# A linear-attention kernel fused with two feed-forward layers: the normed unit is transposed at the end of TensorE's step, the state's sum and decay move in halves

## What is computed

```
scale = min(|a|, 0.999) / (|a| + 1e-6),  a_n = a * scale      (a complex)
S = a_n[t] * S + k[t] v[t]^T ;   y[t] = q[t] . Re S
x  = y, heads side by side: 3072 rows of 384
xn = x / sqrt(mean(x*x) + 1e-6) * g
x2 = (silu(xn @ w_gate) * (xn @ w_val)) @ w_out               (384 -> 1536 -> 384)
out = softplus(x2 @ w_in) @ w_out2                            (384 -> 2048 -> 384)
```

## Time and profile before

| | |
|---|---|
| median of 3 runs | 1287.45 us (1284.30 to 1287.48) |
| profiled execution, its own time | 1289.8 us |
| its span, first to last instruction | 1288.1 us |
| TensorE matmul busy | 1117.6 us (87%), 5495 instructions |
| TensorE weight load busy | 940.5 us (73%) |
| VectorE busy | 751.8 us (58%), 2204 instructions |
| ScalarE busy | 617.9 us (48%) |
| GpSimd busy | 307.4 us (24%) |
| granted TensorE clock, mean | 0.965 of full speed |
| DMA queues, share of 16 engines | 24.2% |

### The profile page before, as it was taken

How to read it: one execution, slowest core, us unless ns; L and a number is a source line. 1 busy time by engine, 2 the same in 40 slices (tenths; PEclk the granted TensorE clock), 3 DMA queues, 4 the chain that set the end, 5 groups by cost and what they waited for, 6 DMA issues and landing times.

```text
span 1288.1 us, 18819 instructions
## 1 busy us (share of the span) xinstructions
PE 1117.6 (87%) x5495; PEld 940.5 (73%) x5495; DVE 751.8 (58%) x2204; ACT 617.9 (48%) x1136; POOL 307.4 (24%) x260
## 2 busy tenths in 40 slices
PE   0444469999999899989898999998999999999996
PEld 0444457777777777777777788887888888888885
DVE  7788878798888798889889841121222222222211
ACT  2233334444444444444444433345666666666664
POOL 0023331111111111111111111464333333333332
PEclk9999998898999899999899899999999999999999
DMA  2444442242333323333332230232010101010000
GB/s 70 118 134 129 130 117 55 75 122 79 88 104 93 91 70 113 91 85 96 95 99 83 68 93 1 77 119 87 1 50 1 50 1 50 0 49 0 24 1 25
DMA packets 63850, 91.22 MB, mean 71 GB/s; under 512 B 4624, under 2 KB 53648, under 8 KB 63760
## 3 DMA queue, kind: packets, MB, share of 16 engines
q1 hardware_dynamic: 63760, 90.15, 24.2%
HBM read 60.89 MB, written 29.24 MB: 70 GB/s over the span
## 4 chain that ended last, share of the span: by engine, by line
issue 30%; PE 26%; DVE 19%; DMA 11%; POOL 9%; SPq 2%; ACT 1%; DVEq 1%; POOLq 0%; ACTq 0%
PE gbank L1303 13%; POOL pl L539 9%; DVE prep L819 8%; DMA rows_scratch<-pk 6%; DMA mm<-rows_scratch 5%; DVE pk L819 4%; PE xbank L1332 3%; PE xbank L1331 3%; PE ybank L1303 3%; PE xbank L1335 2%; SPq L336 1%; DVE xn L1039 1%; PE sbank L1343 1%; DVE state L1002 1%; DVE at L1009 1%
## 5 line engine op out<-in xcount | busy, mean ns | idle before, releaser
L1303 PE MATMUL gbank<-xh,slab 128*128 128x512 f32 x1296 | 426.0, 411 | 1.9 <-issue 1.9
L1303 PE MATMUL ybank<-ph,slab 128*128 128x512 f32 x1020 | 319.2, 394 | 4.9 <-ACT ytile L645 4.0
L1303 PEld LDWEIGHTS gbank<-xh,slab 128*128 128x128 f32 x1296 | 255.4, 200 | 55.1 <-issue 2.1
L1303 PE MATMUL gbank<-xl,slab 128*128 128x512 f32 x648 | 262.2, 405 | 0.0
L514 POOL TENSOR_TENSOR pl<-hid,ph 128x512 fp32r<-128x512 f32 x72 | 107.3, 1490 | 535.9 <-ACT ph L638 535.9
L1303 PEld LDWEIGHTS ybank<-ph,slab 128*128 128x128 f32 x1020 | 189.3, 189 | 43.0 <-issue 5.6
L1303 PE MATMUL ybank<-pl,slab 128*128 128x512 f32 x510 | 199.3, 391 | 0.0
L539 POOL TENSOR_TENSOR pl<-hid,ph 128x512 fp32r<-128x512 f32 x96 | 125.7, 1309 | 267.0 <-ACT ph L756 267.0
L1187 DVE SCALAR_TENSOR_TENSOR hid<-gbank,hid 128x512 f32<-128x512 f32 x72 | 49.8, 691 | 214.4 <-ACT hid L747 214.4
L1303 PEld LDWEIGHTS gbank<-xl,slab 128*128 128x128 f32 x648 | 128.6, 198 | 29.1
L1050 DVE TENSOR_TENSOR hid<-gbank,hid 128x512 f32<-128x512 f32 x72 | 49.7, 691 | 115.7 <-PE gbank L1303 112.8
(11 more groups left out here) (124 smaller groups left out, 1561.9 us busy)
## 6 DMA issues: line engine op xcount, KB each, us to landing
rows_scratch<-pk SPq DMA_DIRECT2D x24, 771.0 KB, 5.0
mm<-rows_scratch SPq DMA_DIRECT2D x96, 192.8 KB, 4.0
a_in<-in_a SPq DMA_DIRECT2D x24, 384.0 KB, 5.3
kq_in<-in_kq SPq DMA_DIRECT2D x24, 384.0 KB, 4.9
ytile<-in_w SPq DMA_DIRECT2D x36, 192.0 KB, 4.3
prep<-in_w SPq DMA_DIRECT2D x32, 192.0 KB, 2.6
y_scratch<-ytile SPq DMA_DIRECT2D x7, 768.0 KB, 5.8
v_in<-in_v SPq DMA_DIRECT2D x24, 192.0 KB, 4.6
```

The source lines that it names most:

```text
L1303: last = pe.matmul(out, slab[:, slot + part, cols], x, start=f, stop=l)
```

## The change

Six edits, on four engines:

1. **TensorE:** `xt_of(x)` moves from before `outputs(m, 0)` to before `outputs(m, 1)`. It now waits for `mask(m, 1)`, and `scores(m, 0)` instead of `scores(m, 1)` waits for `x_low` (of the step before).
2. **ScalarE:** `xh_of` moves to match, from before `y_copy(m, 0)` to before `y_copy(m, 1)`, behind `hi(3i + 2)`. **VectorE:** `x_low` moves from before `p_of(3i + 2)` to just before `keys`.
3. **VectorE:** `decay` is split in halves of four heads. `decay(m, 0)` stands before `total`, `decay(m, 1)` before `scaled_frame`; each waits for its own half of `mm`, and `outputs(m, hf)` for its own half.
4. **VectorE:** `state_add(m, 1)` moves from the end of a step into the next one, behind `limits(n)`.
5. **VectorE:** `p_of(3i + 1)` moves ahead of `mask(m, 0)`, `sum_of(n + 1)` some ten operations forward, `query` ahead of `p_of(3i + 2)`, `mask(m, 1)` ahead of `odd`, and the small operations of the norm one place back each.
6. **SyncE:** `load_a(n + 1)` moves from behind `load_kq(n)` to between the two halves of `load_mm`.

What is stored in `pk`, `mm` and the scratch is the same as before. The core of the diff:

```diff
@@ SyncE, step
                     load_mm(m, 0, 1 - par)
+                if n is not None and not (isinstance(n, int) and n + 1 >= NU):
+                    load_a(n + 1)
+                if m is not None:
                     load_mm(m, 1, 1 - par)
...
                 if w1 is not None:
-                    load_a(n + 1)
                     load_w1(w1 + 1)
@@ ScalarE, step
-                if x is not None:
-                    xh_of(x, par, col, T)
                 if m is not None:
                     y_copy(m, 0)
...
+                if x is not None:
+                    xh_of(x, par, col, T)
                 if m is not None:
                     y_copy(m, 1)
@@ VectorE
-            def decay(m):
-                dve.wait_ge(mm_loaded[0], 32 * (m + 1))
-                dve.wait_ge(mm_loaded[1], 32 * (m + 1))
-                need(dve, s_added, 2 * m)
-                dve.tensor_tensor(state[:, :, :], state[:, :, :],
-                                  mm[:, :, 2 * CH:2 * CH + 1].broadcast_to([2 * D, H, D]), ALU.mult).then_inc(decayed, 1)
+            def decay(m, hf):
+                dve.wait_ge(mm_loaded[hf], 32 * (m + 1))
+                need(dve, s_added, 2 * m + hf - 1)
+                heads = slice(hf * HH, (hf + 1) * HH)
+                dve.tensor_tensor(state[:, heads, :], state[:, heads, :],
+                                  mm[:, heads, 2 * CH:2 * CH + 1].broadcast_to([2 * D, HH, D]), ALU.mult).then_inc(decayed, 1)
@@ TensorE
             def scores(m, hf):
                 need(pe, masked, 2 * m + hf)
-                if hf:
-                    pe.wait_ge(xl_done, m + 1)
+                if not hf:
+                    need(pe, xl_done, m)
...
-                pe.wait_ge(decayed, m + 1)
+                pe.wait_ge(decayed, 2 * m + hf + 1)
...
-                pe.wait_ge(masked, 2 * m + 1 if m is not None else 2 * NU)
+                pe.wait_ge(masked, 2 * (m + 1) if m is not None else 2 * NU)
@@ TensorE, step
-                if x is not None:
-                    xt_of(x, m)
                 if m is not None:
                     outputs(m, 0)
...
                     out_block(T, 3 * i + 2)
+                if x is not None:
+                    xt_of(x, m)
                 if m is not None:
                     outputs(m, 1)
```

More of the change, by code:

```diff
@@ L369, in step @@
                 if w1 is not None:
-                    load_a(n + 1)
                     load_w1(w1 + 1)
                     load_w1(w1 + 2)
-                elif n is not None and not (isinstance(n, int) and n + 1 >= NU):
-                    load_a(n + 1)
                 if n is not None:
@@ L1063, in step @@
                     limits(n)
+                if m is not None and not (isinstance(m, int) and m == 0):
+                    state_add(m - 1, 1)
+                if n is not None:
                     scale(n)
@@ L1078, in step @@
                     total_products(n)
+                if m is not None:
+                    decay(m, 0)
+                if n is not None:
                     total(n)
+                if T is not None:
+                    p_of(T, 3 * i + 1)
+                if n is not None:
                     after_products(n, 1)
@@ L1082, in step @@
                     mask(m, 0)
-                    decay(m)
                 if n is not None:
@@ L1087, in step @@
                     x_mean(x)
-                    x_first(x)
                 if n is not None:
                     after_products(n, 2)
+                if n is not None and not (isinstance(n, int) and n + 1 >= NU):
+                    sum_of(n + 1)
                 if x is not None:
-                    x_second(x)
+                    x_first(x)
                 if n is not None:
@@ L1096, in step @@
                 if x is not None:
-                    x_root(x)
+                    x_second(x)
                 if n is not None:
@@ L1101, in step @@
                 if x is not None:
-                    x_norm(x)
+                    x_root(x)
                 if n is not None:
@@ L1106, in step @@
                     end_root(n)
[L1107 to L1110, removed]
+                if x is not None:
+                    x_norm(x)
                 if n is not None:
@@ L1113, in step @@
                     after_sums(n, 8)
+                if T is not None and i == 0:
+                    y_out(T)
+                if n is not None:
                     turn_of(n)
@@ L1116, in step @@
                     frame_sums(n)
-                if T is not None and i == 0:
-                    y_out(T)
+                if m is not None:
+                    decay(m, 1)
                 if n is not None:
@@ L1123, in step @@
                     carry_of(n)
+                    last(n)
                 if m is not None:
@@ L1126, in step @@
                 if n is not None:
-                    last(n)
                     middle_products(n)
+                    query(n)
                     middle(n)
-                if x is not None:
-                    x_low(x, par, col)
                 if T is not None:
@@ L1135, in step @@
                     odd_products(n)
-                    query(n)
-                    odd(n)
                 if m is not None:
@@ L1140, in step @@
                 if n is not None:
+                    odd(n)
                     even_products(n)
                     even(n)
+                if x is not None:
+                    x_low(x, par, col)
+                if n is not None:
                     keys(n, 0)
@@ L1146, in step @@
                     queries(n, 1)
-                if m is not None:
-                    state_add(m, 1)
             def x2_low(T, par):
```

## The result

| | before | after |
|---|---|---|
| median | 1287.17 us (4 runs, 1284.30 to 1287.48) | 1211.08 us (4 runs, 1208.93 to 1212.67) |
| ratio | | 0.9412, 95% interval 0.9392 to 0.9433 |
| profiled execution, span | 1288.1 us | 1209.8 us |
| granted clock, mean | 0.965 | 0.994 |
| TensorE matmul busy | 1117.6 us | 1080.2 us |

The account below looks back on a forecast made before the run. TensorE was held by waits and a lowered clock, with VectorE the next bound at 28.0 us a lap. Terms summed to -79.6 us from 1289.8, giving 1210.2; less 2.35 for the median, 1208 us, range 1190 to 1240.

Parts of the forecast that it names:

- The wait for `xn` goes, and the clock comes back: TensorE, second stage: wait before the transposes goes, 1.7 us per lap on average; clock gives back up to 41.7 us.
- The first rival: Part is given back: clock still falls once per lap or the square lands no earlier; laps 29.5, 1235 us; chance 0.25.
- VectorE becomes the bound at 28.0 us a lap: Second stage: VectorE's own work 27.6 us, plus 0.06 for split decay and 0.3 of wait, sets the lap.
- the 0.3 us for `sum_of`: VectorE: the earlier sum_of(n + 1) waits 0.3 us per lap for ScalarE's square of a; bounds 0 and 1.8 us.
- TensorE waits 1.3 us for `mm` in each lap: TensorE at kt_of(m, 0): its 26.7 us lap against VectorE's 28.0 leaves a wait of 1.3 us.
- The last unit costs 2 us: Last unit, no attention to follow: transposes come at the step's end and tile 5 waits for copy and remainder, +2 us.
- The first stage: Four laps fall from 32.82 to 28.9 us: both state_add waits go, a wait of 0.8 for mask(m, 0) comes; -15.7 us.
- moves cost nothing by themselves: VectorE: reordering its operations adds no time of its own to the lap; only the second decay instruction adds 0.06 us.
- The wait for mask(m, 0): First stage: scores end 12.5 us after the store, VectorE reaches the mask at 11.8; wait 0.8 us.
- Second stage: 17 laps fall from 31.54 to 28.0 us, 3.54 each; -60.2 us.
- The step before these: Step before the first stage's four laps, without xn: -1.5 us, an estimate from the state_add(m, 1) wait of 1.86.
- From line 828 of unit 23 to the end: Lap of unit 23 -3.5 us, step with attention but no unit to prepare -0.7, last unit +2, third stage 0.

Follow-up runs that it names:

- e1: The kernel before with only the transposes of xn, ScalarE's copy and x_low moved to their new places; 1244.2 us, ratio 0.966.
- e2: The changed kernel with the transposes of xn, ScalarE's copy and x_low put back to their old places; 1332.0 us, ratio 1.033 to the kernel before.
- e8: The changed kernel with TensorE's wait for xn added before outputs(m, 0), transposes staying at the end; 1325.8 us, ratio 1.031 to the kernel before.
- e5: The changed kernel with the load of the next a behind the load of kq again; 1237.0 us, ratio 0.962 to the kernel before.
- e6: The changed kernel with GpSimd splitting only 16 of 384 columns of each first-layer weight; 1205 us, executed once.
- e7: The kernel before with GpSimd splitting only 16 of 384 columns of each first-layer weight; 1286 us, executed once.
- e3: The changed kernel with the decay of all eight heads at once, at the first half's place; 1308.5 us, ratio 1.018 to the kernel before.

## Why the prediction was right

**The wait for `xn` goes, and the clock comes back.** Right. No wait for `xn` is left, the clock is 0.99, and TensorE's busy time is 37 us less, where the prediction had up to 41.7. e1, e2 and e8 bear it out from both sides. The first rival, laps of 29.5 with the clock still falling, did not come in the changed kernel. Its mechanism is not refuted, though: in e1, behind short waits in front of transposes and small matmuls, the clock did fall, 4 times in 17. The sentence of the Trainium skill on transposes ("TensorE: Matmul & The Clock Gate", Part 4: PE-mode transpose), that they do not count as activity the way matmuls do, was the reason given for that rival. The changed kernel has its transposes, 0.49 us, right in front of `outputs(m, 1)` with no wait before them, and the clock stays up; e8 has none at the old place and it falls behind 3 us of wait; e1 has them behind 0.5 to 0.9 us of wait and it falls now and then. No run separates what the transposes add to a wait, so what the page says of them is neither shown nor refuted here. In the changed kernel the two do not meet: no wait stands before the transposes, and none of length before the small matmuls of `outputs`.

**VectorE becomes the bound at 28.0 us a lap.** Right in kind, and the mean is 27.94; that it is so close is in part luck. The forecast was for one lap like the next. Thirteen of the 17 laps are 26.7 to 27.7 us, under the forecast: the 0.3 us for `sum_of` was not there, and VectorE's busy time per lap fell from 27.2 to 26.8 us, where the prediction had it rise by 0.06. Four longer laps, of which the prediction knows nothing, bring the mean up: the first of the stage, and three around 401 us, where TensorE and VectorE stand still for 2.5 and 2.9 us before work for which the profile shows no wait. The trace of the changed kernel shows the loads in the new order, and the square:

```profile
242.28 0.81 SPq L336 DMA_DIRECT2D mm<-rows_scratch  x2
243.36 0.36 SPq L321 DMA_DIRECT2D a_in<-in_a  x1
243.83 0.86 SPq L336 DMA_DIRECT2D mm<-rows_scratch  x2
...
247.56 0.85 ACT L557 ACTIVATE front<-a_in 128x768 f32<-128x768 f32 x1 [0.37 <-DMA a_in<-in_a]
```

The square starts 10.6 us after line 828, where I had estimated 11.8. The load of `a`, issued at 243.36, took 4.2 us to the square and not the 5.77 of before. Over the 17 laps the square starts 11.5 us after line 828 on average, against 13.0 in the kernel before. That 1.5 us matters, as e5 shows. In the prediction's way to mask(m, 0), 257.90 to 268.71 less 0.30 is 10.5 us and not 10.4, which changes nothing.

**TensorE waits 1.3 us for `mm` in each lap.** In direction right, too high: 0.96 us at 246.12, none at 272.49, and 6.7 us in all over the stage, 0.4 per lap. Most laps are also nearer to TensorE's own 26.4 us than forecast.

**The last unit costs 2 us.** Right in kind: one wait at the start of tile 5, where the transposes have no `outputs` behind them.

```profile
724.26 0.70 PE L1312 MATMUL gbank<-xh,slab 128*128 128x512 f32 x2 [1.47 <-ACT xh L611]
```

**The first stage: the term that was mis-sized.** I put its lap at 28.9 us; it is 30.3, and four laps make 5.6 us of the sum. The step that failed is "32.82 - 2.97 - 1.86 + 0.06": it took the waits out and VectorE's work as unchanged but for 0.06 us. The four laps in the kernel before and in the changed one (columns as in the earlier trace rows):

```profile
58.23:189.49 131.26, 64.69 (x303) 60.21 (x304) 108.31 (x334) 46.75 (x113) 40.47 (x36) 1.00 0.46 132
```

```profile
56.19:177.38 121.19, 62.50 (x303) 59.21 (x302) 115.92 (x337) 46.74 (x112) 39.20 (x36) 1.00 0.51 143
```

VectorE is busy 108.31 / 4 = 27.1 us per lap before and 115.92 / 4 = 29.0 us after, 1.9 us more for the same work. The prediction took the 2.97 us of VectorE's wait as empty. In the kernel before, GpSimd's second group of three splits of weights ran in just that time:

```profile
141.64 2.90 POOL L501 TENSOR_TENSOR slab<-ytile,slab 128x384 f32 x3 [8.99 <-ACT slab L617]
```

```profile
139.85 0.17 DVE L819 TENSOR_TENSOR turn<-ga,gv 128x6 f32<-128x6 f32 x1
140.05 0.17 DVE L819 TENSOR_TENSOR cu<-frame,turn 128x6 f32<-128x6 f32 x1
...
140.33 0.23 DVE L819 TENSOR_TENSOR frame<-cu,cw 128x3 f32<-128x3 f32 x2
...
144.35 0.35 DVE L1015 TENSOR_TENSOR state<-xbank,state 96x192 f32<-96x192 f32 x1 [2.97 <-ACT xnat L604]
```

The three splits take 2.90 us from 141.64, VectorE waits until 144.35, and the six-column operations before them take 0.17 us each. In the changed kernel VectorE does not wait there, and the splits fall on those small operations:

```profile
133.57 2.90 POOL L501 TENSOR_TENSOR slab<-ytile,slab 128x384 f32 x3 [6.76 <-ACT slab L617]
```

```profile
129.19 0.69 DVE L1009 TENSOR_TENSOR at<-sbank,causal 128x512 f32<-128x512 f32 x1 [0.68 <-PE sbank L1329]
...
133.61 0.98 DVE L819 TENSOR_TENSOR turn<-ga,gv 128x6 f32<-128x6 f32 x1
134.62 0.91 DVE L819 TENSOR_TENSOR cu<-frame,turn 128x6 f32<-128x6 f32 x1
...
135.65 0.91 DVE L819 TENSOR_TENSOR frame<-cu,cw 128x3 f32<-128x3 f32 x2
```

`turn` takes 0.98 us for its six columns and `cu` 0.91, and the pair `frame` 0.91: some 2.2 us more than the same instructions took before, beside splits from 133.57 to 136.47. With the splits cut to 16 columns they are short again (e6):

```profile
109.22 0.19 DVE L820 TENSOR_TENSOR turn<-ga,gv 128x6 f32<-128x6 f32 x1
109.45 0.17 DVE L820 TENSOR_TENSOR cu<-frame,turn 128x6 f32<-128x6 f32 x1
```

So in this lap a wait of 2.97 us was removed and 2.2 us of stretching came in its place. The Trainium skill ("SBUF — State Buffer", Who interferes with whom) says that the pair of ports that VectorE and GpSimd share is an exclusive lock, and that a VectorE instruction with two inputs in SBUF contends with a GpSimd instruction that reads SBUF. The trace agrees: `turn` and `cu`, with both inputs in SBUF, grow by 0.8 and 0.7 us beside splits of 0.97 us, though they have six columns. The wait for mask(m, 0), 0.68 us in this lap, came as forecast (0.8).

e6 and e7 bear out the cause, not the whole size. With the splits cut, VectorE's busy time is nearly the same in both kernels, 22.5 and 22.7 us per lap, so the 1.9 us are the splits' doing. But other waits grow where the stretching goes (that for the first scores to 2.5 us per lap in e6 and 1.8 in e7), and the gap between the laps grows by 0.8 us only, to 3.3, where the prediction had 3.9.

**The sum.** Second stage: 17 x (31.54 - 27.94) = 61.2 us, forecast 60.2. First: 4 x (32.82 - 30.30) = 10.1, forecast 15.7. The step before these 2.3 (1.5). From line 828 of unit 23 to the end 5.0 us, forecast 2.2; the runs do not tell which term of that is off. The first stage gave 5.6 us less than forecast and the rest some 4.6 us more, so that the profiled execution came to 1211.6 us for a forecast of 1210.2: here misses of opposite sign cancel, which is luck. The other 1.8 us up to the 3 by which the median is off (1211 for 1208) are that it lies 0.5 us under its profiled execution and not 2.35.

**What the prediction did not see** is how closely the edits depend on one another. It costed each move at its own wait. e2 and e8 (3%) and e3 (1.8%) show that VectorE's new order with the old place of the transposes or the old wait, or with the decay in one piece, is slower than the kernel before. The prediction's reading holds for all edits together, in which few waits of TensorE are longer than a microsecond; "moves cost nothing by themselves" does not hold for VectorE's new order without the move of the transposes.

## What to carry to other kernels

When two engines are near the same pace, look at the few waits that one has for the other and at the clock behind them: here 32 us of waits stood beside some 42 us lost to the lower clock. Moving one consumer eight microseconds later removed the waits and most of the clock's loss (0.93 to 0.98 in e1), and the other edits the rest. Before an idle stretch is counted as a gain, look at what the engine's port neighbour does in it; work that ran there unseen may fall on something else. And edits that move work earlier on one engine are safe only if the waits that they make stay short: test them together, not one by one.

## What was not expected of the hardware

- The granted clock fell behind 16 of TensorE's 19 waits for `xn` in the kernel before (1.5 to 2.6 us but for one of 0.5) and at all 15 in e8 (2.2 to 3.4 us), and stayed at the lower level for some 3 to 10 us. It fell behind 4 of 17 waits of 0.5 to 0.9 us before the transposes in e1, and behind none before the transposes of keys in e5 and in the changed kernel, the longest of which were 1.6 and 1.5 us. What work follows a wait seems to count; which part of it does is open. In the changed kernel it fell once, at a wait of 2.49 us for nothing that the profile shows, near 401 us (0.91 from 380 to 420 us).
- 2.5 us more wait on VectorE (e3) made a lap 4.5 us longer: TensorE waited behind it, 2.5 us too, and its clock was 0.91 against 0.99.
- A VectorE operation of six columns took 0.98 us instead of 0.17 beside a GpSimd operation.
